# Ahead tiles of five groups' rows, the first expert's weights split in quarters, and the first group's places two steps sooner, in a convolution and two mixture-of-experts layers

## What is computed

```python
# attention: per head a 7-tap causal convolution with softmax weights
x = attention(x, weight).reshape(N, D)
# first layer: only rows with a positive skip score are computed
do = x @ w_skip > 0
e1 = argmax(x @ w_gate, axis=1)
x[do] = x[do] + gate * (relu(x[do] @ w1[e1]) @ w2[e1])   # the others pass through
# second layer: every row
e2 = argmax(normalised(x) @ normalised(emb).T / tau, axis=1)
out = gate2 * (relu(x @ w1b[e2]) @ w2b[e2])
```

## Time and profile before

| what | value |
|---|---|
| median of 3 runs | 1178.58 us (1177.01 to 1186.67) |
| profiled execution | 1183.37 us, span 1181.7 us |
| TensorE matmul busy | 1111.3 us, 94% of the span |
| VectorE busy | 744.2 us, 63% |
| ScalarE busy | 555.0 us, 47% |
| GpSimd busy | 411.0 us, 35% |
| mean granted TensorE clock | 0.969 |

### The profile page before, as it was taken

How to read it: one execution, slowest core, us unless ns; L and a number is a source line. 1 busy time by engine, 2 the same in 40 slices (tenths; PEclk the granted TensorE clock), 3 DMA queues, 4 the chain that set the end, 5 groups by cost and what they waited for, 6 DMA issues and landing times.

```text
span 1181.7 us, 28316 instructions
## 1 busy us (share of the span) xinstructions
PE 1111.3 (94%) x8229; PEld 1068.9 (90%) x8230; DVE 744.2 (63%) x2136; ACT 555.0 (47%) x1499; POOL 411.0 (35%) x532
## 2 busy tenths in 40 slices
PE   4999979699999999999979999999999999999996
PEld 2777769699998999999879999999999999999995
DVE  2565768667777777778674655656556565565553
ACT  2554624144434343434344655656555565565553
POOL 1077777212212121222223333333333333333333
PEclk9999958799999999999988999999999999999998
DMA  5554355403313032133023131313113113111111
GB/s 153 160 171 153 107 182 169 125 22 104 88 39 97 27 104 85 38 90 102 23 95 90 41 103 43 101 44 95 50 33 109 39 31 110 41 40 41 41 41 34
DMA packets 62986, 96.28 MB, mean 81 GB/s; under 512 B 9235, under 2 KB 49898, under 8 KB 62816
## 3 DMA queue, kind: packets, MB, share of 16 engines
q1 hardware_dynamic: 43040, 48.85, 14.5%
q0 software_dynamic: 19904, 46.89, 12.9%
HBM read 61.21 MB, written 36.05 MB: 82 GB/s over the span
## 4 chain that ended last, share of the span: by engine, by line
PE 75%; DVE 8%; issue 6%; POOL 4%; DMA 2%; DVEq 1%; SPq 1%; ACT 1%; POOLq 0%
PE ph L1069 34%; PE py L1080 22%; PE py L1085 10%; POOL bucket_rows L1438 4%; PE pt L1057 2%; PE pt L1058 2%; PE ph L1660 1%; PE ph L1661 1%; DVE w1s L420 1%; DVE h_lo L833 1%; DMA bucket_rows<-xrow,idx_row 1%; PE pu L1112 1%; DVE y_sum L893 1%; PE pu L1110 1%; PE pu L1111 1%
## 5 line engine op out<-in xcount | busy, mean ns | idle before, releaser
L1080 PE MATMUL py<-w2s,h_hi 128*128 128x384 f32 x1472 | 443.4, 365 | 0.6
L1069 PE MATMUL ph<-xa_hi,w1s 128*128 128x256 f32 x1472 | 392.6, 288 | 17.7 <-issue 16.0
L594 ACT ACTIVATE h_hi<-ph 128x512 fp32r<-128x512 f32 x368 | 218.0, 593 | 330.5 <-PE ph L1069 328.7
L1085 PE MATMUL py<-w2s,h_lo 128*128 128x192 f32 x1472 | 347.2, 256 | 1.9 <-DVE h_lo L833 1.8
L833 DVE SCALAR_TENSOR_TENSOR h_lo<-ph,h_hi 128x512 fp32r<-128x512 f32 x368 | 249.8, 689 | 140.2 <-ACT h_hi L594 136.7
L1069 PEld LDWEIGHTS ph<-xa_hi,w1s 128*128 128x128 f32 x1472 | 283.3, 192 | 19.3 <-issue 17.0
L1069 PE MATMUL ph<-xb,w1s 128*128 128x256 f32 x1472 | 297.2, 283 | 0.0
L1085 PEld LDWEIGHTS py<-w2s,h_lo 128*128 128x128 f32 x1472 | 280.2, 192 | 2.4 <-issue 2.4
L1080 PEld LDWEIGHTS py<-w2s,h_hi 128*128 128x128 f32 x1472 | 272.2, 190 | 2.0 <-issue 2.0
L1069 PEld LDWEIGHTS ph<-xb,w1s 128*128 128x128 f32 x1472 | 229.8, 192 | 0.0
L1069 PE MATMUL ph<-xa_lo,w1s 128*128 128x256 f32 x736 | 208.9, 284 | 0.0
(11 more groups left out here) (248 smaller groups left out, 1475.0 us busy)
## 6 DMA issues: line engine op xcount, KB each, us to landing
xg<-bucket_rows POOLq DMA_DIRECT2D x89, 202.0 KB, 2.7
w2raw<-in_moe_w SPq DMA_DIRECT2D x16, 768.0 KB
w1raw<-in_moe_w SPq DMA_DIRECT2D x16, 512.0 KB
w1raw<-in_moe_w SPq DMA_DIRECT2D x32, 256.0 KB
work<-in_x SPq DMA_DIRECT2D x4, 1440.0 KB
work<-in_x SPq DMA_DIRECT2D x4, 1344.0 KB
bucket_rows<-fill SPq DMA_DIRECT2D x24, 202.0 KB, 2.4
out_rows<-work,idx_tok POOLq DMA_INDIRECT x118, 2.4
```

Source lines behind the costliest of these rows:

```text
L594: act.activation(h_hi[:, 2 * q:2 * q + 2, :], ph[q][:, :].rearrange("p (c t) -> p c t", c=2), ACT.Relu).then_inc(layers[l]["h_high"], 1)
L1069: ins = pe.matmul(to, w, v[:, :], start=n == 0, stop=n == len(parts) - 1)
L1080: return pe.matmul(py[s][:, 0:2 * D], h_hi[:, f, t], w2s[:, slot, f, :, :].rearrange("p c d -> p (c d)"), start=f == 0, stop=f == FC - 1)
L1085: return pe.matmul(py[s][:, 0:D], h_lo[:, f, t], w2s[:, slot, f, 0, :], start=False, stop=False)
```

## The change

Three things are changed together. `TAIL` goes from 2 to 3, so the ahead tiles hold rows of five groups instead of six, and `ahead_dve` runs in group 5 instead of group 6. The split of expert 0's weights is cut into four quarters: ACT takes them at steps 4 and 6 of groups 4 and 5, DVE at steps 3 and 5 of groups 5 and 6. And for the first group's routing, which is done in group 1, `step_of` gives other steps: `mark_codes` at step 0, `mark_buckets` and the exponentials at step 1, `positions` and `place` at step 2.

```diff
@@ -62,7 +62,7 @@
 
     AHEAD = ((0, 0), (0, 1), (1, 0), (1, 1))
     NA = len(AHEAD)
-    TAIL = 2
+    TAIL = 3
     FIRST = 2
     NTILES = (N + EARLY * TILE) // TILE + E
     assert NA == FIRST * SUB and NA % 2 == 0
@@ -313,6 +313,7 @@
         e_pad = sem("early_padding_stored")
         w_raw = sem("weights_loaded")
         w_hi = sem("weights_high")
+        w_half = sem("second_weights_half_high")
         w_one = sem("first_weights_split")
         w_ready = sem("weights_split")
         WP = 3
@@ -327,6 +328,11 @@
         block = ctx.enter_context(nc.Block())
 
         BLOCK = 8
+
+        def step_of(g, k):
+
+
+            return max(k - 1, 0) if g == 1 and k < 4 else k - 2 if g == 1 else k
 
         AHEAD_AT = 512 - SUB
         ALL = 256
@@ -372,7 +378,8 @@
 
         NW = 4
 
-        WEIGHTS = 6
+        HIGH_AT = ((4, 4), (4, 6), (5, 4), (5, 6))
+        LOW_AT = ((5, 3), (5, 5), (6, 3), (6, 5))
 
         def load_group(sp, g):
             b, part = divmod(g, GPB)
@@ -411,6 +418,33 @@
         def split_high(act, slot):
             split_high1(act, slot)
             split_high2(act, slot)
+
+        def split_high_quarter(act, q):
+
+            t1, t2 = slots(0)
+            c = slice(q % 2 * (FC // 2), (q % 2 + 1) * (FC // 2))
+            if q < 2:
+                act.activation(t1[:, 0, q, :], w1raw[:, q, :], ACT.Copy).then_inc(w_hi, 1)
+            elif q == 2:
+                act.activation(t2[:, c, 0, :], w2raw[:, c, :], ACT.Copy).then_inc(w_half, 1)
+            else:
+                act.activation(t2[:, c, 0, :], w2raw[:, c, :], ACT.Copy).then_inc(w_hi, 1)
+
+        def split_low_quarter(dve, q):
+            t1, t2 = slots(0)
+            c = slice(q % 2 * (FC // 2), (q % 2 + 1) * (FC // 2))
+            if q < 2:
+                dve.wait_ge(w_hi, q + 1)
+                ins = dve.tensor_tensor(t1[:, 1, q, :], w1raw[:, q, :], t1[:, 0, q, :].bitcast(fp32), ALU.subtract)
+                if q == 1:
+                    ins.then_inc(w_one, 1)
+            elif q == 2:
+                dve.wait_ge(w_half, 1)
+                dve.tensor_tensor(t2[:, c, 1, :], w2raw[:, c, :], t2[:, c, 0, :].bitcast(fp32), ALU.subtract)
+            else:
+                dve.wait_ge(w_hi, WP)
+                dve.tensor_tensor(t2[:, c, 1, :], w2raw[:, c, :], t2[:, c, 0, :].bitcast(fp32),
+                                  ALU.subtract).then_inc(w_ready, 1)
 
         def split_low1(dve, slot, expert):
 
@@ -1481,11 +1515,12 @@
                     if g + 1 < NG:
                         evacuate(g + 1, k)
                     copy(g, k)
-                    if k == 2 and g > 0:
+                    if k == step_of(g, 2) and g > 0:
                         exponentials(g - 1)
-                    if g == WEIGHTS and k == 2:
-                        act.wait_ge(w_raw, 16 * NW)
-                        split_high(act, 0)
+                    if (g, k) in HIGH_AT:
+                        if (g, k) == HIGH_AT[0]:
+                            act.wait_ge(w_raw, 16 * NW)
+                        split_high_quarter(act, HIGH_AT.index((g, k)))
                 if g + 1 < NG:
                     evacuate(g + 1, STEPS)
 
@@ -1619,18 +1654,17 @@
                     if k == 0 and g > 0:
                         route = Chain(dve, a_rt, (g - 1) * ROUTE)
                         mark_scores(g - 1, route)
-                    if k == 1 and g > 0:
+                    if k == step_of(g, 1) and g > 0:
                         mark_codes(g - 1, route)
-                    if k == 2 and g > 0:
+                    if k == step_of(g, 2) and g > 0:
                         mark_buckets(g - 1, route)
-                    if k == 4 and g > 0:
+                    if k == step_of(g, 4) and g > 0:
                         if g - 1 == NG - 1 - TAIL:
                             dve.wait_ge(a_pos, g)
                             ahead_dve(dve)
                         place(g - 1)
-                    if g == WEIGHTS and k == 5:
-                        split_low1(dve, 0, 0)
-                        split_low2(dve, 0, 0)
+                    if (g, k) in LOW_AT:
+                        split_low_quarter(dve, LOW_AT.index((g, k)))
             route = Chain(dve, a_rt, (NG - 1) * ROUTE)
             mark_scores(NG - 1, route)
             x_low(dve, 0, 1)
```

## The result

| | before | after |
|---|---|---|
| median of 4 runs | 1177.8 us (1176.88 to 1186.67) | 1197.2 us (1193.95 to 1202.33) |
| profiled execution | 1183.37 us, span 1181.7 us | 1194.49 us, span 1192.9 us |
| mean granted clock | 0.969 | 0.969 |

The ratio is 1.015, with a 95% interval of 1.0124 to 1.0176. By the ratio the change makes the kernel some 18 us slower. 1186.5 was forecast, with 1193 as the upper end, so the time lies outside the range. So what the two traces show is a little more than half of it.

What follows compares the result with a forecast made beforehand. TensorE, near full clock almost everywhere, was taken as the bound, with GpSimd's scatters a chain as long as its attention phase. Front -3.1 and tile +11.0 gave +7.9 us, 1191.3, scaled to 1186.5; range 1178 to 1193.

Steps and rivals of the forecast that it cites:

- The tile: In the loop, padding of expert 0's ahead tiles makes a 34th tile that nothing hides: +11.0 us.
- The stall in group 1: TensorE waits 3.8 us at the first positions, plus 2.5 of half clock; GpSimd starts group 1 4.9 us later.
- R1: Rival: no long stall in group 1, the front gives 8.5 to 10 us, time 1180.3; chance 0.16.
- The quarters: Splitting the weights in quarters cuts TensorE's wait near 150 us by 3.6; the full clock in group 7 brings 2.9.
- the first product: The ahead tiles' first product on TensorE starts 2.9 us sooner than 177.59, at about 175.
- R2: Rival: the clock doesn't hold in group 7, the front gives about 0, time 1189.6; chance 0.16.
- 2.05 us too much to 0.8: GpSimd's scatter issues slowed beside the split lose 0.8 instead of 2.05 us, a gain of 1.2.
- the term of -8.4 us: Quarters, clock, the load's wait and smaller waits together start the first product 8.4 us sooner, before the later GpSimd.
- Tile 2's places, which it waits for at 217.29, come at 212.4: After tile 0, TensorE's 4.9 us gain carries through to tile 2's places, which GpSimd awaits.
- the gather at 216.4: GpSimd's gather of the loop's first tile comes at about 216.4 instead of 219.53: -3.1 us for the front.
- R4: Rival: the stall spreads to VectorE's and ScalarE's turns, GpSimd ends after 215, front loses 3 us, 1192.6; chance 0.13.
- R3: Rival: no 34th tile, so the front's gain alone stands, time 1175.5; chance 0.05.

Runs made afterwards that it cites:

- pad20_again: Kernel before with 20 padding places counted as taken in the ahead tiles, making 34 tiles, on a full-clock chip: 1.009, +10.6 us.
- the two exchanges: Experts 0 and 1 exchanged with 2 and 3, giving 33 tiles, in the changed kernel and in it with the old steps: 1.0091 and 1.0028.
- swap_old_steps: Changed kernel with the first group's routing at its old steps and experts 0 and 1 exchanged with 2 and 3 (33 tiles): 1.0028.
- after_again: The changed kernel, unchanged, timed and traced again on another full-clock chip: 1199.59 us, 1.0163 against the kernel before.
- swap_after: Changed kernel with experts 0 and 1 exchanged with 2 and 3 in the first layer, giving 33 tiles: 1.0091 against the kernel before.
- same_again: The kernel before, unchanged, traced a second time: 1184.61 us in the traced execution, on a chip with a median of 1181.15.
- the hold: SyncE loads expert 2's weights only once the loop's first gather has landed, in the kernel before and the changed kernel: 1.0005 and 1.0119.
- old_steps: Changed kernel with the first group's routing back at its old steps, five groups and quarters kept, 34 tiles: 1.0098 against the kernel before.
- hold_before: Kernel before with SyncE's load of expert 2's weights held until the loop's first gather has landed, on a slower chip: 1.0005.
- steps_only: Kernel before with only the first group's routing two steps sooner, 33 tiles, on a slower chip: 1.0017.

## Why the prediction was wrong

**The tile: right.** +11.0 us was forecast. On chips A pad20_again has 10.6 us for it, and the two exchanges 8.3 and 8.5. One step of the loop was mis-sized. Between the loop's second tile and the second layer's first tile, evacuations of the transposed rows on ScalarE, the kernel before:

```profile
244.15 0.38 ACT L589 ACTIVATE xa_hi<-pt 128x256 fp32r<-128x256 f32 x1
...
568.93 0.38 ACT L589 ACTIVATE xa_hi<-pt 128x256 fp32r<-128x256 f32 x1
```

324.78 us. After, and then swap_old_steps:

```profile
248.03 0.38 ACT L623 ACTIVATE xa_hi<-pt 128x256 fp32r<-128x256 f32 x1
...
581.81 0.38 ACT L623 ACTIVATE xa_hi<-pt 128x256 fp32r<-128x256 f32 x1
```
```profile
248.42 0.38 ACT L623 ACTIVATE xa_hi<-pt 128x256 fp32r<-128x256 f32 x1
...
573.64 0.38 ACT L623 ACTIVATE xa_hi<-pt 128x256 fp32r<-128x256 f32 x1
```

333.78 and 325.22 us: the tile costs 9.0 and 8.6 us there, not 11.0. The same stretch of pad20_again is 577.94 - 244.01 = 333.93. The rest of its 10.6 must lie outside this stretch. With 34 tiles the odd tile's code is jumped over, and TensorE stands 3.23 us at 590.25 with nothing to wait for in the profile (3.0 to 3.4 in four traces with 34 tiles; with 33 it waits 2.4 to 2.5 us for VectorE's counts at about that place). That the jump is the cause was not tested. From the second layer's first tile to the second layer's loop takes 58.4 to 64.3 us in the traces with 34 tiles and 58.0 to 61.2 in those with 33.

**The stall in group 1: right, and what follows it at least as large as forecast.** TensorE stands 3.80 us at the positions, as worked out, with the clock at 0.50 behind it. GpSimd's group 1 starts 2.7 us later by the traces' clocks, but 4.6 when the earlier start of this execution is taken out, 4.7 in after_again and 7.0 in swap_after, where 4.9 was forecast. R1 falls.

**The quarters: wrong twice, and it did not show in the first product.** The clock does not hold in group 7, which is R2's mechanism. And the slower issues do not go from 2.05 us too much to 0.8: the mean of all 112 rose from 1005 to 1022 ns, 1.9 us together, with single issues of 2.03 and 1.90 where the earlier trace rows had 1.50 and 2.50. In the trace of after, VectorE's quarter at 128.88 ends at 130.11 and GpSimd's issue at 130.96; all four issues that begin beside a quarter end 0.84 or 0.85 us after it, and so does the issue of 2.50 us of before. So an issue that meets an instruction of the split ends at a fixed time after that instruction, wherever in it it began. The Trainium skill's rule (SBUF — State Buffer, "SBUF: two separate sides"), that a DMA issued from GpSimd is locked out while VectorE has the port pair they share, would have given no gain here. The section states that lock for VectorE's 2-port modes, and for an instruction with two SBUF inputs, as the split is, only against a GpSimd operation that reads SBUF. The trace agrees with the lock-out, and has a small loss besides, 1.9 us against the first trace of before and 1.0 against the second.

The first product at 174.70, where 174.7 was forecast, is luck. The 1.9 us of earlier start are in it; measured from the evacuation the first product is 1.0 us sooner than before, in after_again 1.2 us later than in same_again, in swap_after 2.3 us later than before, where 2.9 sooner was forecast. The end of the scatters at 211.24, where 211.0 was forecast, has the same luck: it is 6.7 us later than before, not 4.6. With the old steps the first product is 174.27, so the term of -8.4 us was -3.3.

**The step that failed is in the sum: "Tile 2's places, which it waits for at 217.29, come at 212.4", and the gather at 216.4.** It took TensorE's 4.9 us at tile 0 through to tile 2's places. But these are made in the buffer that row 0's scatters read, and those are behind the whole chain of GpSimd, which ends 4.9 us later. An earlier TensorE runs into a later GpSimd: 6.10 us of wait on VectorE, places at about 220.3, the gather at 222.80. Every trace of five groups on a chip A in which row 0 is not issued sooner has this wait, 3.30 to 6.10 us, and no trace of six groups there has it. The forecast had GpSimd's end as a floor for the gather by its 5.1 us of issues alone, and not by what its landing frees. In both traces of after the loop's first tile is late, by 2.6 us (225.67 against 223.06) and by 5.0 (228.09), where -3.1 was forecast: 5.7 to 8.1 of the 11 us that the forecast is short. Also the gather's own time was taken as fixed. It lands 2.9 us after its issue at 222.80 and 6.0 at 222.09, 7.4 at 217.94 and 7.3 at 219.83. From the end of GpSimd's row scatters to TensorE's going on it is 14.4 to 17.5 us in the traces of chips A, and 11.5 and 11.8 in the two with row 0 sooner, so that is no fixed time either. What sets the gather's landing was not settled. The early tiles' rows and expert 2's weights keep the DMA engines busy in the same microseconds, which fits, but the hold that was to test it ran only where they don't meet.

**What adds up and what stays open.** On chips A: tile 10.6, the two other edits 1.0 (1.0098 against 1.009, within the error), steps 7.7, together 19.2 us, the 1.0163 of after_again, as it must be with differences of the same ratios. They are of two chips of the kind. The steps' 7.4 to 7.7 us are in the traces of the swapped pair too: 7.4 us at the end of the scatters and 7.3 at the loop's first tile. Between after and old_steps it is 3.4 and 0.3 there, but these two traces lie on the wrong sides of their medians. And the medians are 18.4 to 19.4 us apart where the first pair of traces is 11.1. Of the difference 1.9 us is the earlier start. swap_after shows one thing that can make an execution of the changed kernel longer, the 1.2 GHz lasting 10 us and not 7; whether it is that in the executions without a trace is open.

One number of the range does not follow: R1's better end, with 10 us from the front, is 1179.6 and not 1178. Nothing hangs on it.

**The rivals.** R2's mechanism happened, with the tile and the stall as forecast. R4's time is the nearest. Its condition, that GpSimd ends 8.6 us later or more, is not met in the first trace (4.9, or 6.7 from the evacuation) nor in after_again, but it is in swap_after (9.2 from the evacuation, 7.4 of it by the steps). So R4 may hold in some executions and is not out. R3 and R1 are.

## What to carry to other kernels

When a stage is made to start sooner, ask of every buffer it writes who read it last and when that reader's transfer lands: if that reader is queued behind the chain you have just lengthened, the early start is given back there, and once that is mended the next transfer behind the same chain takes it. Count whole tiles with the data before splitting a bucket: 68 padding rows cost one tile of 8 to 11 us on chips A, more than the 3.1 us that all else here was forecast to bring. And before a reordering puts a wait ahead of independent work in a dense in-order queue, price the wait and the clock behind it: here 3.80 us of stall with 7 to 10 us at 1.2 GHz, and 7.4 to 7.7 us in the medians.

## What was not expected of the hardware

- The same kernel takes 1178 to 1181 us on some chips and 1248 to 1255 us on others, and nearly all of it is there before the loop: hold_before comes to the loop's first tile at 282.94 and the kernel before on a chip A at 223.06, 59.9 of the 62.5 us between their executions. In that stretch hold_before's granted clock is 0.50 to 0.83 over windows from 70 to 250 us, where the other has 1.00 up to 150. TensorE also waits more there, and which causes which was not tested. The loop stretch runs alike on both, 346.0 us with 33 tiles (steps_only) beside 345.2 (before). A tile cost 9.2 and 16.6 us on chips B, 8.3 to 10.6 on A. The quarters help on chips B, 0.9967 and 0.9962; on chips A, together with five groups, they bring nothing.
- A gather of one tile landed 2.9 to 7.4 us after its issue. The nearer it was to SyncE's weight loads, with the DMA engines busy, the longer it took.
- An indirect DMA's issue on GpSimd that began during one of VectorE's subtractions of 128x768 to 128x1536 fp32 elements ended 0.84 or 0.85 us after it: 1.09 to 2.50 us in place of 0.97.
- TensorE stood 3.0 to 3.4 us with nothing to wait for in the profile where it had the odd tile's code to jump over.
